# Attention work and weight splits rearranged over ACT, DVE and POOL in a fused attention and feed-forward kernel

## The chip, the cores and the metric

The kernel runs on one core of one Trainium2 chip. The metric is the device time of the whole program in microseconds (us), median of several runs; lower is better. The engines are named as the profile names them: PE (TensorE, matmuls), DVE (VectorE), ACT (ScalarE), POOL (GpSimd) and SP (SyncE, which here issues all DMAs).

## What is computed

Inputs are q, k, v of shape (4 batches, 8 heads, 576 tokens, 64 columns) and two pairs of weights, each w_in (512 x 2048) and w_out (2048 x 512), all fp32. The reference, cut to what matters:

```python
q_d, k_d, v_d = (t.reshape(B, H, S // 4, 4, D).mean(axis=3) for t in (q, k, v))
out_up = np.repeat(softmax(scale * q_d @ k_d.T) @ v_d, 4, axis=2)
mask = np.abs(pos[:, None] - pos[None, :]) < 4
out_local = softmax(np.where(mask, scale * q @ k.T, -1e9)) @ v
x = (out_up + out_local).transpose(0, 2, 1, 3).reshape(B * S, H * D)
h = x @ w_in1;  x = np.maximum(0.01 * h, h) @ w_out1       # 2304 tokens x 512
h = x @ w_in2;  out = (h - np.tanh(h)) @ w_out2
```

Both softmaxes subtract the row maximum and add 1e-9 to the row sum. The first attention works on means over four tokens ("downsampled"), the second only in a band of seven keys around each token ("local").

## The kernel before

**Matmuls.** Each fp32 matmul of the two feed-forward layers is done as three fp32r matmuls: an operand is split into a rounded part (`_hi`, a copy by ACT) and the rest (`_lo = raw - hi`, a subtraction by DVE or POOL), and hi*hi, hi*lo and lo*hi are summed in PSUM. All weights, all x and all g (the hidden activations) are split that way.

**Stages.** Heads are worked in 16 pairs. `batch0` computes the first four pairs (two in the buffers A, two in the buffers B) and four steps of the next. Then come eight tiles of layer 1 of 288 tokens each. The first six are "mixed": between the matmuls of a tile the engines do the steps of two more pairs of heads in the buffers A. The last two have layer 1 alone. Then follow six tiles of layer 2 of 384 tokens.

**Steps of a pair.** A pair takes 17 steps, one per slot. In batch0 pair A stands at step `slot % 17` and pair B five slots behind; in a mixed tile slot s runs step `(s + 4) % 17`. Steps 0 and 1: PE turns q, and the two halves are copied from PSUM into `q_diag` (ACT copies the one of step 0, DVE the one of step 1). Steps 2 and 3: the same for k into `kT`. Steps 3 and 4: DVE sums groups of four of both (the means). Steps 4 and 5: local scores, DVE adds the band. Step 5: POOL sums v over groups of four (`vd`, L970, three instructions), for which v must have been loaded. Step 6: DVE takes the local row maximum and subtracts it. Step 7: DVE takes the maximum of the downsampled scores (L814) and subtracts it (L816); ACT takes exp of the local scores (L588). Step 8: ACT takes exp of the downsampled scores `pd` (L591); DVE sums the local rows, adds 1e-9, inverts and multiplies `pl` by the inverse (L829). Step 9: DVE sums the downsampled rows (L835), adds 1e-9 and inverts. Step 10: POOL multiplies `pd` by the inverse (L977). Steps 11 to 14: PE turns `pl` and `pd`, ACT copies them out. Steps 15 and 16: PE multiplies with v, DVE combines both into xT (L765).

**Layer 1.** A tile runs over 16 chunks f of 128 hidden columns. PE computes `hidden1(f)`, then `down1(f - 2)`. ACT takes 0.01*h (L658), DVE the maximum (g, L871), ACT `g_hi` (L640), DVE `g_lo` (L856), and `down1(f)` waits for `g_lo(f)`. The weights of chunks 0 to 7 (`w_hi_a`, `w_lo_a`) are split once and kept: `split_kept(f)` is one ACT copy of 128 x 1024 (L616) and one POOL subtraction of the same size (L983). Before the change all eight are done in batch0, at the slots of `KEPT_SLOTS`. `hidden1(f)` waits for `kept_lo_done >= f + 1`. The weights of chunks 8 to 15 stay whole in `w_whole` and are split again in every tile (`in_hi`/`out_hi` by ACT, L624 and L628; `in_lo`/`out_lo` by POOL, L988 and L993). In the first tile of layer 1, ACT waits at chunk 6 for `whole_loaded`.

**Orders.** Every engine runs its own list of instructions in order. In batch0 the two pairs of a slot are sorted so that the one at a step under 6 comes first. In a mixed tile POOL's list for chunk f is `split_out(f-1)`, slot 2f, `split_in(f+2)`, slot 2f+1. ACT's is `split_out(f-1)`, leak(f), `g_hi(f-1)`, slot 2f, `split_in(f+2)`, slot 2f+1. DVE's is g(f), `g_lo(f-1)`, slot 2f, slot 2f+1. SP issues the loads in one order written out by hand, with waits in between: `load_qk(s, i)` waits for PE's step 3 of the pair before in the same buffers, `load_v(s, i)` for its step 16, `load_kept(f)` for `kept_lo_done >= f - 3`, since four slots of `w_whole` serve the kept weights in turn. The last four chunks of `w_whole` use the same four slots and are loaded when the kept ones there have been split.

Of the kernel before, what the change touches and what calls it, by code (L numbers as in the profile page):

```python
# [31 lines left out]
P = 128  # L32
# [8 lines left out]
KEPT_SLOTS = (9, 12, 17, 20, 25, 28, 33, 36)  # L41
# [16 lines left out]
def two_scale_attention_and_feed_forward(nc, q, k, v, w_in1, w_out1, w_in2, w_out2, out):  # L58
# [11 lines left out]
    SCALE = float(D) ** -0.5  # L70
    PAIRS = B * H // 2
# [9 lines left out]
    WHOLE = CF - KEPT  # L81
    assert D == QB and DM == CD * P and LP * RUN == S and NB * QB == S and PAIRS == 4 + 2 * MIXED

# [8 lines left out]
    with ExitStack() as ctx:  # L92
# [6 lines left out]
        def sem(name):  # L99
            return ctx.enter_context(nc.semaphore(name))  # L100
# [25 lines left out]
        class PairBuffers:  # L126

            def __init__(self, which, place, banks):
# [18 lines left out]
                self.exp_l, self.exp_d = sem(f"exp_l_{which}"), sem(f"exp_d_{which}")  # L147
                self.sum_l, self.sum_d = sem(f"sum_l_{which}"), sem(f"sum_d_{which}")
# [49 lines left out]
        whole_loaded = sem("whole_loaded")  # L198
# [19 lines left out]
        def uses0(i, n):  # L218


            return 7 * i + n
# [47 lines left out]
        def _(sp):  # L269
# [32 lines left out]
            def load_whole(j):  # L302
                if j >= WHOLE - 4:
                    sp.wait_ge(kept_lo_done, j - (WHOLE - 4) + KEPT - 3)
                load_w(w_whole[:, j, :], 0, KEPT + j, whole_loaded)
# [4 lines left out]
            load_kept(0)  # L310
            load_kept(1)
            load_qk(A, 1, 2)
            load_kept(2)
            load_kept(3)
            load_kept(4)
            load_qk(B, 1, 6)
            load_kept(5)
            load_v(A, 1, 2)
            load_kept(6)
            load_qk(A, 2, 8)  # L320
            load_kept(7)
            load_v(B, 1, 6)
            for j in range(WHOLE - 4):
                load_whole(j)
            load_v(A, 2, 8)
            for j in range(WHOLE - 4, WHOLE):
                load_whole(j)
            load_qk(A, 3, 10)
            load_v(A, 3, 10)
# [245 lines left out]
        def _(act):  # L575
            def attention(step, s, i):
                if step == 0:
                    act.wait_ge(s.bank_full[1], uses1(i, 1))
                    for h in range(2):
                        rows = slice(h * D, (h + 1) * D)  # L580
                        last = act.activation(q_part(s, rows, h, 0), token_part(s, rows, 0), ACT.Copy)
                    last.then_inc(s.bank_free[1], 1)
                elif step == 2:
                    act.wait_ge(s.bank_full[1], uses1(i, 2))
                    act.activation(k_part(s, 0), k_tokens(s, 0), ACT.Copy).then_inc(s.bank_free[1], 1)
                elif step == 7:
                    act.wait_ge(s.sub_l, i + 1)
                    act.activation(s.pl[:, :, :], s.pl[:, :, :], ACT.Exp, scale=SCALE).then_inc(s.exp_l, 1)  # L588
                elif step == 8:
                    act.wait_ge(s.bank_free[0], uses0(i, 4))  # L590
                    act.activation(s.pd[:, :, :], s.pd[:, :, :], ACT.Exp, scale=SCALE / FACTOR ** 2).then_inc(s.exp_d, 1)  # L591
# [26 lines left out]
            def split_in(tile, f):  # L618

                if f == KEPT:  # L620
                    act.wait_ge(whole_loaded, 32 * WHOLE)

                wait_from(act, h_done, CF * tile + (f - 1 if f >= KEPT + 2 else 0))
                act.activation(in_hi[:, f % 2, :], w_whole[:, f - KEPT, 0:DM], ACT.Copy).then_inc(in_hi_done, 1)  # L624
# [23 lines left out]
            def layer1(tile, between, extra, keep_before, ahead):  # L648
                for f in range(CF + 1):
                    n = CF * tile + f  # L650
                    if f == CF:
                        ahead()
                    if f - 1 >= KEPT:
                        split_out(tile, f - 1)
# [106 lines left out]
        def _(dve):  # L761
# [8 lines left out]
            def attention(step, s, i, batch, c):  # L770

                if step == 1:
                    dve.wait_ge(s.bank_full[0], uses0(i, 1))
                    for h in range(2):
                        rows = slice(h * D, (h + 1) * D)
                        last = dve.tensor_copy(q_part(s, rows, h, 1), token_part(s, rows, 1))
                    last.then_inc(s.bank_free[0], 1)
                elif step == 3:
                    dve.wait_ge(s.bank_full[0], uses0(i, 2))
                    dve.tensor_copy(k_part(s, 1), k_tokens(s, 1)).then_inc(s.bank_free[0], 1)  # L780

# [29 lines left out]
                elif step == 7:  # L811
                    dve.wait_ge(s.bank_full[0], uses0(i, 4))
                    quarter = s.banks[0:QP, 0, 0:QT * SD_].rearrange("p (t k) -> p t k", t=QT)
                    dve.tensor_reduce(s.mxd[:, :], quarter, AX_X, ALU.max).then_inc(s.max_d, 1)  # L814
                    dve.wait_ge(s.max_d, i + 1)
                    dve.tensor_tensor(s.pd[:, :, :], quarter,  # L816
                                      s.mxd[:, :].rearrange("p (t o) -> p t o", o=1).to_broadcast([QP, QT, SD_]),
                                      ALU.subtract).then_inc(s.bank_free[0], 1)
                elif step == 8:
# [8 lines left out]
                    dve.wait_ge(s.inv_l, i + 1)  # L828
                    dve.tensor_tensor(s.pl[:, :, :], s.pl[:, :, :],  # L829
                                      row_l.rearrange("p (n o) -> p n o", o=1).to_broadcast([P, NB, WIN]),  # L830
                                      ALU.mult).then_inc(s.norm_l, 1)
                elif step == 9:
                    row_d = s.rs[0:QP, NB:NB + QT]
                    dve.wait_ge(s.exp_d, i + 1)
                    dve.tensor_reduce(row_d, s.pd[:, :, :], AX_X, ALU.add).then_inc(s.sum_d, 1)  # L835
                    dve.wait_ge(s.sum_d, i + 1)
# [124 lines left out]
        def _(pool):  # L961
            def attention(step, s, i):
                if step == 5:
# [10 lines left out]
                    ins.then_inc(s.vd_done, 1)  # L974
                elif step == 10:
# [20 lines left out]
            def layer1(tile, between):  # L996
                for f in range(CF + 1):
                    if f - 1 >= KEPT:
                        split_out(tile, f - 1)
# [35 lines left out]
            hidden_score = -1e9 * float(D) ** 0.5  # L1035
# [56 lines left out]
```

## Time and profile before

| what | value |
|---|---|
| median of 3 runs | 1017.73 us (1016.67 to 1022.43) |
| span of the profiled execution | 1015.2 us |
| time of the profiled execution itself | not listed apart from its span |
| batch0 | from 0 to about 77 us |
| six mixed tiles | about 69.9 us each |
| mean granted clock of PE over the span | 0.986 |

A row of a timeline gives the start in us from the span's start, the duration in us, the engine, the line of the kernel, the operation, the tile written and the tiles read, the shape, the count, and in brackets how long the engine sat idle before and what ended that. Tiles of pair B stand in the trace under `xT` (as they lie in unused parts of it), `kT_b`, `qn_b`, `kn_b` and `acc`.

### The profile page before, as it was taken

Reading aid. Unit: us, or ns where it says so; the run is one execution under the profiler, and the core shown is the slowest. Engines: PE = TensorE matmul, PEld = TensorE weight load, DVE = VectorE, ACT = ScalarE, POOL = GpSimd, SP = SyncE. Lnnn points to the kernel's source line nnn. Section 1 sums busy time; section 2 is a strip of 40 time slices with the busy share of each in tenths; the row PEclk is TensorE's granted clock in tenths of the full one; section 3 lists DMA queues with packets and bytes.
Section 4 is the critical chain, followed back from the end, with each engine's and each line's share of the span. In section 5 each row is a group of like instructions: output and inputs, shape, how many; then the busy total and the mean of one; then the engine's idle time right before and its main releaser. Section 6 shows DMA issues by size and latency. Waiting matters only on the chain.

```text
span 1015.2 us, 19106 instructions
## 1 busy us (share of the span) xinstructions
PE 964.9 (95%) x6672; PEld 904.3 (89%) x6672; DVE 650.8 (64%) x1178; ACT 538.8 (53%) x1254; POOL 392.4 (39%) x325
## 2 busy tenths in 40 slices
PE   6679999999999999999999999999999999999997
PEld 6568989999899899899999998889899899898996
DVE  7775665864774676658423667677676676666764
ACT  2443443544534534435334667776575675766664
POOL 2651550631723515516234456633333233233232
PEclk9968999999999999999999999999999999999999
DMA  5863211121012012110100402200000000000000
GB/s 130 203 165 97 48 40 31 28 49 26 21 47 47 19 28 47 37 26 11 64 1 1 134 2 63 74 32 1 1 32 0 2 29 0 31 0 0 32 1 32
DMA packets 87221, 41.47 MB, mean 41 GB/s; under 512 B 59776, under 2 KB 80768, under 8 KB 87168
## 3 DMA queue, kind: packets, MB, share of 16 engines
q1 hardware_dynamic: 87168, 40.78, 15.2%
q8 instruction: 32, 0.52, 0.2%
q14 instruction: 21, 0.17, 0.1%
HBM read 36.04 MB, written 4.72 MB: 40 GB/s over the span
## 4 chain that ended last, share of the span: by engine, by line
PE 75%; DVE 9%; SPq 3%; ACT 3%; POOL 3%; issue 3%; DMA 3%; ACTq 0%; DVEq 0%
PE ph L458 12%; PE ph L460 11%; PE ph L459 11%; PE acc L534 6%; PE acc L535 6%; PE acc L536 6%; PE acc L487 6%; PE acc L489 5%; PE acc L488 5%; DVE g_lo L856 4%; PE banks L368 2%; PE banks L386 2%; POOL g_lo L1016 1%; POOL w_lo_b L1023 1%; DVE x_lo L851 1%
## 5 line engine op out<-in xcount | busy, mean ns | idle before, releaser
L1016 POOL TENSOR_TENSOR g_lo<-scratch,g_hi 128x384 fp32r<-128x384 f32 x96 | 126.0, 1312 | 258.9 <-ACT g_hi L640 258.9
L871 DVE TENSOR_TENSOR g<-g,ph 128x288 f32<-128x288 f32 x128 | 57.8, 452 | 161.1 <-ACT g L658 161.1
L988 POOL TENSOR_TENSOR in_lo<-w_whole,in_hi 128x512 fp32r<-128x512 f32 x64 | 88.0, 1375 | 177.2 <-ACT in_hi L624 177.2
L658 ACT ACTIVATE g<-ph 128x288 f32<-128x288 f32 x128 | 52.5, 410 | 192.1 <-PE ph L460 166.0
L458 PE MATMUL ph<-x_hi,w_hi_a 128*128 128x288 f32 (+1 forms) x448 | 144.9, 323 | 3.9 <-DVE x_lo L851 3.9
L460 PE MATMUL ph<-x_hi,w_lo_a 128*128 128x288 f32 (+1 forms) x448 | 140.6, 314 | 0.0
L459 PE MATMUL ph<-x_lo,w_hi_a 128*128 128x288 f32 (+1 forms) x448 | 140.5, 314 | 0.0
L907 DVE SCALAR_TENSOR_TENSOR scratch<-scratch,ph 128x384 f32<-128x384 f32 x96 | 53.2, 554 | 111.0 <-ACT scratch L703 106.4
L993 POOL TENSOR_TENSOR out_lo<-w_whole,out_hi 128x512 fp32r<-128x512 f32 x64 | 87.5, 1368 | 52.7 <-ACT out_hi L628 52.2
L702 ACT ACTIVATE scratch<-ph 128x384 f32<-128x384 f32 x96 | 46.8, 488 | 108.3 <-PE ph L460 106.8
L856 DVE TENSOR_TENSOR g_lo<-g,g_hi 128x288 fp32r<-128x288 f32 x128 | 100.0, 781 | 1.8 <-ACT g_hi L640 1.8
L487 PE MATMUL acc<-g_hi,out_hi 128*128 128x288 f32 x256 | 78.8, 308 | 13.8 <-DVE g_lo L856 13.7
L458 PEld LDWEIGHTS ph<-x_hi,w_hi_a 128*128 128x128 f32 x448 | 84.7, 189 | 8.0 <-issue 3.6
L459 PEld LDWEIGHTS ph<-x_lo,w_hi_a 128*128 128x128 f32 x448 | 84.8, 189 | 1.4
L460 PEld LDWEIGHTS ph<-x_hi,w_lo_a 128*128 128x128 f32 x448 | 84.8, 189 | 0.0
L458 PE MATMUL ph<-x_hi,in_hi 128*128 128x288 f32 x256 | 78.9, 308 | 0.0
L487 PE MATMUL acc<-g_hi,w_hi_a 128*128 128x288 f32 x256 | 78.7, 307 | 0.0
L489 PE MATMUL acc<-g_hi,out_lo 128*128 128x288 f32 x256 | 76.2, 298 | 0.0
L488 PE MATMUL acc<-g_lo,out_hi 128*128 128x288 f32 x256 | 76.0, 297 | 0.0
L459 PE MATMUL ph<-x_lo,in_hi 128*128 128x288 f32 x256 | 75.7, 296 | 0.0
L488 PE MATMUL acc<-g_lo,w_hi_a 128*128 128x288 f32 x256 | 75.6, 295 | 0.0
L489 PE MATMUL acc<-g_hi,w_lo_a 128*128 128x288 f32 x256 | 75.5, 295 | 0.0
(168 smaller groups left out, 2729.1 us busy)
## 6 DMA issues: line engine op xcount, KB each, us to landing
out_dram<-o_stage SPq DMA_DIRECT2D x18, 256.0 KB, 2.1
w_whole<-in_moe_w_in_dram SPq DMA_DIRECT2D x16, 256.0 KB, 4.5
w_whole<-in_moe_w_out_dram SPq DMA_DIRECT2D x16, 256.0 KB, 4.5
qn<-in_q_dram SPq DMA_DIRECT2D x28, 144.0 KB
kn<-in_k_dram SPq DMA_DIRECT2D x28, 144.0 KB
v4n<-in_v_dram SPq DMA_DIRECT2D x28, 144.0 KB
vw<-in_v_dram SPq DMA_DIRECT2D x28, 122.5 KB
scratch<-in_moe_w_in_dram SPq DMA_DIRECT2D x8, 256.0 KB, 3.0
```

Of the source, the lines that this page charges most:

```text
L458: pe.matmul(bank, whi, x_hi[:, c, 0:width], start=(c == 0), stop=False)
L459: pe.matmul(bank, whi, x_lo[:, c, 0:width], start=False, stop=False)
L460: last = pe.matmul(bank, wlo, x_hi[:, c, 0:width], start=False, stop=(c == CD - 1))
L487: pe.matmul(acc[:, c, 0:T1], whi, g1_hi[:, f % 3, :], start=(f == 0), stop=False)
L488: pe.matmul(acc[:, c, 0:T1], whi, g1_lo[:, f % 3, :], start=False, stop=False)
L489: last = pe.matmul(acc[:, c, 0:T1], wlo, g1_hi[:, f % 3, :], start=False, stop=(f == CF - 1))
L534: pe.matmul(acc[:, j, 0:DM], hi, whi, start=(f == 0), stop=False)
L535: pe.matmul(acc[:, j, 0:DM], hi, wlo, start=False, stop=False)
L856: dve.tensor_tensor(g1_lo[:, f % 3, :], g1[:, f % 2, :], g1_hi[:, f % 3, :].bitcast(F32), ALU.subtract).then_inc(g_lo_done, 1)
L988: pool.tensor_tensor(in_lo[:, f % 2, :], w_whole[:, f - KEPT, 0:DM], in_hi[:, f % 2, :].bitcast(F32), ALU.subtract).then_inc(in_lo_done, 1)
L993: pool.tensor_tensor(out_lo[:, f % 2, :], w_whole[:, f - KEPT, DM:CW], out_hi[:, f % 2, :].bitcast(F32), ALU.subtract).then_inc(out_lo_don ...
L1016: pool.tensor_tensor(g2_lo[:, f % 3, :], g2[:, f % 2, :], g2_hi[:, f % 3, :].bitcast(F32), ALU.subtract).then_inc(g_lo_done, 1)
```

## The change

Five edits, made together:

- `KEPT_SLOTS` shrinks from eight slots to (20, 25): batch0 does `split_kept` of chunks 0 and 1 only. Chunks 2 to 7 are done in the first tile of layer 1, by ACT and POOL, `split_kept(f + 2)` at the head of the list of chunk f, for f = 0 to 5.
- SP's order of loads changes: the q, k and v of the next pairs come ahead of weight loads, `kept(6)` and `kept(7)` behind the first four whole chunks, and the last four whole chunks behind q, k and v of pair A 3. They get a semaphore of their own (`rest_loaded`), for which ACT waits at chunk 10 of the first tile; `whole_loaded` now stands for the first four.
- ACT does all four copies of q and k; the scale is folded into them, and the exps and the hidden score change accordingly.
- The downsampled subtraction and row sums leave DVE: DVE takes the negated maximum, and ACT runs three exps of 96 x 144 straight from PSUM with it as bias, each with its row sum accumulated.
- The local normalisation (128 x 630) moves from DVE, step 8, to POOL, step 9.

```diff
-KEPT_SLOTS = (9, 12, 17, 20, 25, 28, 33, 36)
+KEPT_SLOTS = (20, 25)
...
+    Q_SCALE, K_SCALE = SCALE / FACTOR, 1.0 / FACTOR
+    L_SCALE = SCALE / (Q_SCALE * K_SCALE)
...
+    EARLY = len(KEPT_SLOTS)
...
-                load_w(w_whole[:, j, :], 0, KEPT + j, whole_loaded)
+                load_w(w_whole[:, j, :], 0, KEPT + j, whole_loaded if j < WHOLE - 4 else rest_loaded)
...
             load_kept(0)
+            load_qk(A, 1, 2)
             load_kept(1)
-            load_qk(A, 1, 2)
+            load_qk(B, 1, 6)
             load_kept(2)
+            load_v(A, 1, 2)
             load_kept(3)
+            load_v(B, 1, 6)
+            load_qk(A, 2, 8)
             load_kept(4)
-            load_qk(B, 1, 6)
             load_kept(5)
-            load_v(A, 1, 2)
-            load_kept(6)
-            load_qk(A, 2, 8)
-            load_kept(7)
-            load_v(B, 1, 6)
+            load_v(A, 2, 8)
             for j in range(WHOLE - 4):
                 load_whole(j)
-            load_v(A, 2, 8)
+            load_kept(6)
+            load_kept(7)
+            load_qk(A, 3, 10)
+            load_v(A, 3, 10)
             for j in range(WHOLE - 4, WHOLE):
                 load_whole(j)
-            load_qk(A, 3, 10)
-            load_v(A, 3, 10)
...
+                elif step == 1:
+                    act.wait_ge(s.bank_full[0], uses0(i, 1))
+                    for h in range(2):
+                        rows = slice(h * D, (h + 1) * D)
+                        last = act.activation(q_part(s, rows, h, 1), token_part(s, rows, 1), ACT.Copy, scale=Q_SCALE)
+                    last.then_inc(s.bank_free[0], 1)
...
+                elif step == 3:
+                    act.wait_ge(s.bank_full[0], uses0(i, 2))
+                    act.activation(k_part(s, 1), k_tokens(s, 1), ACT.Copy, scale=K_SCALE).then_inc(s.bank_free[0], 1)
...
-                    act.wait_ge(s.bank_free[0], uses0(i, 4))
-                    act.activation(s.pd[:, :, :], s.pd[:, :, :], ACT.Exp, scale=SCALE / FACTOR ** 2).then_inc(s.exp_d, 1)
+                    act.wait_ge(s.max_d, i + 1)
+                    for t in range(QT):
+                        last = act.activation(s.pd[:, t, :], s.banks[0:QP, 0, t * SD_:(t + 1) * SD_], ACT.Exp,
+                                              bias=s.mxd[:, t:t + 1], accum_out=s.rs[0:QP, NB + t:NB + t + 1])
+                    last.then_inc(s.bank_free[0], 1)
...
                 if f == KEPT:
-                    act.wait_ge(whole_loaded, 32 * WHOLE)
+                    act.wait_ge(whole_loaded, 32 * (WHOLE - 4))
+                if f == CF - 4:
+                    act.wait_ge(rest_loaded, 32 * 4)
...
+                    if isinstance(tile, int) and tile == 0 and EARLY <= f + 2 < KEPT:
+                        split_kept(f + 2)
...
-                    dve.tensor_reduce(s.mxd[:, :], quarter, AX_X, ALU.max).then_inc(s.max_d, 1)
-                    dve.wait_ge(s.max_d, i + 1)
-                    dve.tensor_tensor(s.pd[:, :, :], quarter,
-                                      s.mxd[:, :].rearrange("p (t o) -> p t o", o=1).to_broadcast([QP, QT, SD_]),
-                                      ALU.subtract).then_inc(s.bank_free[0], 1)
+                    dve.tensor_reduce(s.mxd[:, :], quarter, AX_X, ALU.max, negate=True).then_inc(s.max_d, 1)
...
-                    dve.wait_ge(s.inv_l, i + 1)
-                    dve.tensor_tensor(s.pl[:, :, :], s.pl[:, :, :],
-                                      row_l.rearrange("p (n o) -> p n o", o=1).to_broadcast([P, NB, WIN]),
-                                      ALU.mult).then_inc(s.norm_l, 1)
...
-                    dve.wait_ge(s.exp_d, i + 1)
-                    dve.tensor_reduce(row_d, s.pd[:, :, :], AX_X, ALU.add).then_inc(s.sum_d, 1)
-                    dve.wait_ge(s.sum_d, i + 1)
+                    dve.wait_ge(s.bank_free[0], uses0(i, 4))
...
+                elif step == 9:
+                    pool.wait_ge(s.inv_l, i + 1)
+                    pool.tensor_tensor(s.pl[:, :, :], s.pl[:, :, :],
+                                       s.rs[:, 0:NB].rearrange("p (n o) -> p n o", o=1).to_broadcast([P, NB, WIN]),
+                                       ALU.mult).then_inc(s.norm_l, 1)
...
+                    if isinstance(tile, int) and tile == 0 and EARLY <= f + 2 < KEPT:
+                        split_kept(f + 2)
...
-            hidden_score = -1e9 * float(D) ** 0.5
+            hidden_score = -1e9 / L_SCALE
```

The DVE copies of q and k (steps 1 and 3 there) go out. Layer 2, the two unmixed tiles and PE's own list stay as they were.

## Rows read from the trace of the kernel before

**Rows 1.** The page's first part: PE's busy time, share of the span, instructions.

```profile
PE 964.9 (95%) x6672; PEld 904.3 (89%) x6672; DVE 650.8 (64%) x1178; ACT 538.8 (53%) x1254; POOL 392.4 (39%) x325
```

**Rows 2.** Windows over the first, second and last mixed tile: length, busy by engine, PEclk, DMA.

```profile
76.00:147.00 71.00, 66.68 (x571) 64.60 (x568) 43.00 (x79) 31.52 (x77) 26.21 (x23) 0.96 0.25 61
147.00:217.00 70.00, 67.56 (x585) 65.34 (x584) 45.53 (x84) 31.77 (x78) 27.47 (x24) 1.00 0.15 36
...
427.00:497.00 70.00, 67.56 (x568) 65.37 (x567) 44.94 (x83) 30.41 (x74) 27.29 (x24) 0.98 0.11 28
```

**Rows 3.** Timeline of SP's DMA queue in batch0: start, time to issue.

```profile
16.75 3.20 SPq L291 DMA_DIRECT2D xT<-in_v_dram  x1
...
37.38 0.81 SPq L282 DMA_DIRECT2D v4n<-in_v_dram  x1
...
45.66 1.64 SPq L273 DMA_DIRECT2D qn<-in_q_dram  x2
...
50.22 0.34 SPq L282 DMA_DIRECT2D xT<-in_v_dram  x1
...
52.34 3.77 SPq L291 DMA_DIRECT2D xT<-in_v_dram  x1
```

**Rows 4.** Timeline of POOL in batch0.

```profile
26.48 2.35 POOL L983 TENSOR_TENSOR w_lo_a<-w_whole,w_hi_a 128x1024 fp32r<-128x1024 f32 x1 [6.48 <-ACT w_hi_a L616]
28.80 2.31 POOL L970 TENSOR_TENSOR xT<-xT 72x256 f32<-72x256 f32 x3
...
60.02 2.32 POOL L970 TENSOR_TENSOR xT<-xT 72x256 f32<-72x256 f32 x3 [5.74 <-DMA xT<-in_v_dram]
62.30 0.90 POOL L977 TENSOR_TENSOR pd<-pd,rs 96x432 f32<-96x432 f32 x1
63.16 2.35 POOL L983 TENSOR_TENSOR w_lo_a<-w_whole,w_hi_a 128x1024 fp32r<-128x1024 f32 x1
```

**Rows 5.** Timeline of DVE in batch0: a local normalisation, and the last combine.

```profile
61.93 4.26 DVE L829 TENSOR_TENSOR xT<-xT 128x630 f32<-128x630 f32 x1
...
76.39 0.69 DVE L765 TENSOR_TENSOR xT<-acc,xT 128x512 f32<-128x512 f32 x1 [0.95 <-PE acc L386]
```

**Rows 6.** Groups by line and shape, whole span: count, busy us, mean ns, idle before.

```profile
L983 POOL TENSOR_TENSOR w_lo_a<-w_whole,w_hi_a 128x1024 fp32r<-128x1024 f32 x8 | 18.9, 2360 | 16.1 <-ACT w_hi_a L616 16.1
...
L776 DVE COPY q_diag<-banks 64x288 f32<-64x288 f32 x28 | 12.7, 454 | 11.3 <-PE banks L362 11.1
L977 POOL TENSOR_TENSOR pd<-pd,rs 96x432 f32<-96x432 f32 x14 | 12.7, 906 | 74.8 <-DVE rs L839 74.8
...
L816 DVE TENSOR_TENSOR pd<-banks,mxd 96x432 f32<-96x432 f32 x14 | 8.4, 603 | 0.5
L616 ACT ACTIVATE w_hi_a<-w_whole 128x1024 fp32r<-128x1024 f32 x8 | 8.4, 1052 | 6.7 <-DMA w_whole<-in_moe_w_out_dram 6.7
...
L611 ACT ACTIVATE up<-banks 128x144 f32<-128x144 f32 x14 | 4.1, 292 | 13.2 <-PE banks L394 12.6
```

**Rows 7.** Timelines of PE and DVE in the first mixed tile.

```profile
90.85 0.29 PE L487 MATMUL acc<-g_hi,w_hi_a 128*128 128x288 f32 x1
...
94.83 0.38 PE L487 MATMUL acc<-g_hi,w_hi_a 128*128 128x288 f32 x1
...
91.52 0.82 DVE L829 TENSOR_TENSOR pl<-pl,rs 128x630 f32<-128x630 f32 x1
```

**Rows 8.** Timelines of DVE, POOL and PE late in the second mixed tile.

```profile
194.81 1.95 DVE L829 TENSOR_TENSOR pl<-pl,rs 128x630 f32<-128x630 f32 x1
...
199.43 4.71 DVE L856 TENSOR_TENSOR g_lo<-g,g_hi 128x288 fp32r<-128x288 f32 x1
...
196.04 1.86 POOL L988 TENSOR_TENSOR in_lo<-w_whole,in_hi 128x512 fp32r<-128x512 f32 x1
...
202.57 1.25 POOL L993 TENSOR_TENSOR out_lo<-w_whole,out_hi 128x512 fp32r<-128x512 f32 x1
...
204.29 0.37 PE L487 MATMUL acc<-g_hi,out_hi 128*128 128x288 f32 x1 [1.71 <-DVE g_lo L856]
```

More of the change, by code:

```diff
@@ L146, in __init__ @@
                 self.means_done, self.sub_l = sem(f"means_done_{which}"), sem(f"sub_l_{which}")
-                self.exp_l, self.exp_d = sem(f"exp_l_{which}"), sem(f"exp_d_{which}")
-                self.sum_l, self.sum_d = sem(f"sum_l_{which}"), sem(f"sum_d_{which}")
+                self.exp_l, self.sum_l = sem(f"exp_l_{which}"), sem(f"sum_l_{which}")
                 self.eps_l, self.eps_d = sem(f"eps_l_{which}"), sem(f"eps_d_{which}")
@@ L580, in attention @@
                         rows = slice(h * D, (h + 1) * D)
-                        last = act.activation(q_part(s, rows, h, 0), token_part(s, rows, 0), ACT.Copy)
+                        last = act.activation(q_part(s, rows, h, 0), token_part(s, rows, 0), ACT.Copy, scale=Q_SCALE)
                     last.then_inc(s.bank_free[1], 1)
+                elif step == 1:
[4 more added lines that the diff above has]
+                    last.then_inc(s.bank_free[0], 1)
                 elif step == 2:
                     act.wait_ge(s.bank_full[1], uses1(i, 2))
-                    act.activation(k_part(s, 0), k_tokens(s, 0), ACT.Copy).then_inc(s.bank_free[1], 1)
+                    act.activation(k_part(s, 0), k_tokens(s, 0), ACT.Copy, scale=K_SCALE).then_inc(s.bank_free[1], 1)
+                elif step == 3:
+                    act.wait_ge(s.bank_full[0], uses0(i, 2))
+                    act.activation(k_part(s, 1), k_tokens(s, 1), ACT.Copy, scale=K_SCALE).then_inc(s.bank_free[0], 1)
                 elif step == 7:
                     act.wait_ge(s.sub_l, i + 1)
-                    act.activation(s.pl[:, :, :], s.pl[:, :, :], ACT.Exp, scale=SCALE).then_inc(s.exp_l, 1)
+                    act.activation(s.pl[:, :, :], s.pl[:, :, :], ACT.Exp, scale=L_SCALE).then_inc(s.exp_l, 1)
                 elif step == 8:
-                    act.wait_ge(s.bank_free[0], uses0(i, 4))
-                    act.activation(s.pd[:, :, :], s.pd[:, :, :], ACT.Exp, scale=SCALE / FACTOR ** 2).then_inc(s.exp_d, 1)
+                    act.wait_ge(s.max_d, i + 1)
[3 more added lines that the diff above has]
+                    last.then_inc(s.bank_free[0], 1)
                 elif step == 11:
@@ L770, in attention @@
             def attention(step, s, i, batch, c):
[L772 to L780, printed above, removed]
+                if step == 3:
                     dve.wait_ge(s.bank_free[1], uses1(i, 1))
```

2 lines of the change are left out of this document (1 added, 1 removed).

## The prediction

> **What bounds the kernel now.** I read the page first: PE is busy 95% of the span [rows 1], so time can only come from places where PE is not fed, and the rest of the chip matters where it feeds PE. Then the windows by stage. A mixed tile lasts 70 us and PE is busy 67.56 of them [rows 2]; 2.4 us a tile is nearly all there is to win in these six. The two unmixed tiles and layer 2 are not touched by the change. That leaves batch0, the stage before the first tile, where PE has little work and a chain through all engines sets the pace; it ends with the last combine, at 76.39 + 0.69 us [rows 5]. Then the timelines. In batch0 the reader should look at what POOL waits for: at 26.48 it has stood 6.48 us for a weight split behind ACT, which itself waited for weights from DRAM, and the sum of v (L970) that stands behind it in POOL's list starts only at 28.80; at 60.02 it has stood 5.74 us for v of pair B 1 [rows 4]. In the late mixed tile the reader should look at two durations: `g_lo` took 4.71 us, and PE stood 1.71 us for it [rows 8].
>
> The second point carries most of what follows. Uncontended, DVE's 128x630 product of two SBUF operands takes 0.82 us [rows 7]. At 194.81 it took 1.95 and ended when a POOL instruction had ended; POOL's next one (196.04) then took 1.86 for its usual 1.3, as it waited in its turn [rows 8]. The `g_lo` that started at 199.43 ended 0.3 us after POOL's instruction of 202.57 to 203.82, and in batch0 the one of 61.93 took 4.26 and ended 0.7 us after POOL's weight split of 63.16 to 65.51 [rows 4, 5, 8]. So such a DVE instruction and a POOL instruction exclude each other, and a POOL queue whose instructions are all ready is not interrupted: DVE waits for the queue, not for one instruction. DVE instructions that read PSUM (L816, the copies) show no such wait.
>
> The Trainium skill (SBUF — State Buffer, section "Who interferes with whom") says that a DVE instruction with two SBUF inputs contends with a POOL instruction that reads SBUF, and that the loser blocks until the first has finished. The trace agrees with the exclusion; the 4.71 us goes past one instruction, where by the page's rule it would be 1.7 at most. What that rule would do to the time is the first rival.
>
> **Part 1, batch0.** Removed there: six of eight weight splits, 2.36 us of POOL and 1.05 of ACT each [rows 6]. On the path is the one of 26.48. With it gone the v sum of pair B 0 waits only for its load: issued until 16.75 + 3.20 = 19.95, and landing as the later one did, 60.02 - (52.34 + 3.77) = 3.9 us after the issue [rows 3, 4], so at 23.9 instead of 28.8. That is -4.9; I take -4.4, because the POOL normalisation comes in. PE's step 16 of pair A 0, and SP's load of v of A 1 at 37.38 that waits for it [rows 3], come earlier by that. Next, v of B 1: before, SP issues v of A 1, kept(6), q and k of A 2, kept(7), and gets to it at 50.22, 12.84 us after 37.38. Now only v of A 1 and kept(3) stand between, which take what v of A 1 and kept(6) took, 45.66 - 37.38 = 8.3 us [rows 3]. That is another -4.5, -9 in all at 60.02. POOL's `pd` product at 62.30 follows, and from it the chain to the combine at 76.39 is copies and transposes: 14 us, as before. Two ACT splits of 1.05 leave it, and a second q and k copy (0.454 each for 288 columns on DVE [rows 6], and there are three a pair, which ACT now does one after the other) come in: -2.1 + 1.4, about -0.5. The DVE work removed (per pair three copies of 0.454, the subtraction of 0.603 [rows 6], a sum of about the same, the product of 0.82 [rows 7]: 3.4 us) shortens a busy engine, but the v of B 1 is then what is late, so I count nothing more for it. Sum: **-9.4**, bounds -4 (only the first wait goes; the rest comes back on the chain through ACT) and -13 (the removed DVE work of one pair shows too).
>
> **Part 2, the first tile.** The six splits land on POOL and ACT while PE is fed by DVE. ACT's copy for weight chunk 4 stands ahead of leak(2), and POOL's 2.36 us then run just when `g_lo(1)` is due; PE wanted it at 90.85 [rows 7]. ACT's 1.05 is also ahead of it: PE waits about 2.5 us. Behind `g_lo(1)` DVE sums and inverts the local rows, about 1.3 us; POOL multiplies, 1.3 to 1.45 us (0.906 x 630/432 by the `pd` product, 2.36 x 630/1024 by the split [rows 6]), where DVE took 0.82; PE's turn of `pl` waits another 1.2. Then POOL's queue has no hole: product 1.4, split 5 2.36, `pd` 0.91, split 6 2.36, together 7.0 us [rows 6], and `g_lo(2)` asks for its turn in it. PE, now 3.7 late, wants it at 94.83 + 3.7 = 98.5 [rows 7] and gets it near 101.5: 3 more. Sum 6.7, and I take **+6** as ACT runs a little ahead in places; bounds +2.5 (only the first wait) and +10 (with a fall of the clock, below). SP's part: kept(6) and kept(7) are issued once splits 2 and 3 are done, some 15 us before their use; the last whole chunks are issued after v of A 3, whose wait ends near chunk 6, and need about 4 us for v, 5.5 for the four loads and 3.9 to land, while chunk 10 comes some 18 us later. I cost both at nothing; the margin is about 4 us.
>
> **Part 3, the rest of the mixed tiles.** Per tile: in the first half POOL's product takes 0.5 to 0.6 more than DVE's 0.82 and PE's turn stands right behind it; after some slack +0.3 (bounds 0, +0.6). In the second half the DVE instruction of 194.81 goes and POOL gets 1.4 us between its splits. POOL's queue at 194.8 then runs without a hole through `out_lo`, the product and `in_lo` (4.0 us), so `g_lo(10)` comes about 0.8 later than now, and the next, that of 199.43 [rows 8], meets the same queue of `pd`, `out_lo`, `in_lo`, `out_lo`. It comes out between 1.0 earlier, if the last of these loses its turn because ACT is late with its copy, and 0.3 later. At the tile's end ACT's second q copy (2 x 0.45) delays `x_hi` by about 1 us, while the later `out_lo` leaves `x_lo` alone: 0 to +0.2. I take +0.3 a tile, times 6: **+2**, bounds -4 and +14. The three exps of 144 columns cost ACT 3 x 0.292 = 0.9 [rows 6] for one exp of about 0.6; it lies beside POOL and PE work. Of these I know no row with a row sum accumulated; at twice the price, 1.8, `leak(11)` and with it `g_lo(10)` would come 0.9 later.
>
> **Sum.** -9.4 + 6 + 2 = -1.4 us, made against the span of 1015.2; the median of the runs is 2.5 above that span, and I carry the difference over: 1017.7 - 1.4 = **1016.3**. What a measurement of this kernel can tell from no change is 0.5%, 5.1 us.
>
> **Clock.** The first tile's window has a mean clock of 0.96 and the last one's 0.98 [rows 2]: 0.02 x 70 is 1.4 us, one short fall to half (1.2 GHz) after the wait for `g_lo`, absent in the second tile with the same wait. Part 2's waits are longer, so one or two such falls are likely there, 1.4 us each at least; this is in the bounds, not in the sum.
>
> **Rivals.**
> (a) DVE gets its turn after each POOL instruction, as at 194.81 [rows 8]. Then part 2 is +2.5 and part 3 about -0.4 a tile, -2.5: -9.4 + 2.5 - 2.5 gives 1008.3. For it: that row, and the skill's rule named above. Against it: 4.71 and 4.26 us. Chance 0.32 (with a batch0 gain at its upper bound beside it).
> (b) Slower: in each mixed tile ACT's k copy (0.45) delays `in_hi(10)`, POOL's v sums slip, and `in_lo(11)` is then ready before they end, so that POOL runs `in_lo` and `out_lo` on without letting `g_lo(8)` in, 2.6 us more; all behind it slips, and PE loses about 2 a tile. Six tiles: -9.4 + 6 + 14 gives 1028. It decides from 1.1 us a tile on. Against it: the three v sums wait for each other, a hole in which DVE can enter. Chance 0.16.
> (c) Batch0 gives 4, not 9: its end is set by copies in a row on ACT, not by loads. -4 + 6 + 2 gives 1021.7. Chance 0.08.
> (d) The last weights come late, and ACT stands at chunk 10: 5 us past the margin would give 1021. Chance 0.04.
> The forecast itself: 0.40, own range 1012.7 to 1022.5.
>
> Faster by over 0.5%: (a) and a little of the forecast, 0.34. Within: the rest of the forecast, (c) and (d) nearly whole, 0.46. Slower: (b) and the edge of (c) and the forecast, 0.20. The range, 1006 to 1026, leaves out most of (b) and the far end of (a).
>
> **What the profile after would show.** Batch0's last combine at 67 +/- 2, POOL's v sums near 24 and 51. In the first tile waits of PE (L487) on DVE `g_lo` at chunks 3 and 4, of 2.5 and 3 us, with DVE instructions of 2.5 and 6 us beside a closed row of POOL instructions. In the second tile PE's idle time within 1 us of 2.4, again at `g_lo`. Wrong if: a mixed tile changes by over 1 us, if batch0 ends after 73, or if PE stands for `kept_lo` or ACT for a load.

## The result, and the profile after

The changed kernel takes 1002.15 us (median of 4 runs, 1001.27 to 1004.44), the one before 1017.4 beside it (4 runs): ratio 0.984 [0.982, 0.986], 1.6% faster. The prediction was 1016.3 with a range from 1006 to 1026, so the time lies 4 us under the range. The profiled execution's span fell from 1015.2 to 999.6 us.

The page's first part after answers to [rows 1]:

```profile
PE 965.1 (97%) x6672; PEld 906.1 (91%) x6672; DVE 585.8 (59%) x1082; ACT 565.8 (57%) x1382; POOL 410.4 (41%) x341
```

PE's work is the same; it stands idle 15.8 us less (34.5 for 50.3 of the span). To see where, I cut both traces at the first DVE `x_lo` of every tile, where a tile starts. Before, these are at 78.0, 146.7, 216.6, 286.5, 356.5, 426.4 and 495.8, after at 71.2, 141.3, 209.9, 278.3, 346.7, 415.1 and 480.8:

| stretch | before | after | difference |
|---|---|---|---|
| up to the first tile | 78.0 | 71.2 | -6.8 |
| first mixed tile | 68.7 | 70.1 | +1.4 |
| second to fifth, each | 69.9 | 68.4 to 68.6 | -5.9 in all |
| sixth | 69.4 | 65.8 | -3.6 |
| all the rest | 519.4 | 518.8 | -0.6 |

Windows cut at these points, over the first, second and sixth tile, first of the kernel before and then of the kernel after (columns as in [rows 2]):

```profile
78.00:146.70 68.70, 66.02 (x561) 64.13 (x562) 42.00 (x77) 30.73 (x75) 24.75 (x21) 0.97 0.23 54
146.70:216.60 69.90, 67.47 (x584) 65.24 (x584) 45.43 (x82) 31.67 (x77) 27.47 (x24) 1.00 0.15 36
...
426.40:495.80 69.40, 66.96 (x564) 64.83 (x563) 44.34 (x81) 29.81 (x72) 27.48 (x24) 0.98 0.10 23
```

```profile
71.20:141.30 70.10, 66.53 (x564) 64.56 (x565) 38.92 (x66) 38.40 (x93) 42.48 (x31) 0.98 0.39 106
141.30:209.90 68.60, 67.32 (x586) 65.36 (x585) 36.34 (x71) 35.24 (x93) 29.58 (x26) 1.00 0.15 36
...
415.10:480.80 65.70, 64.71 (x560) 62.71 (x559) 36.14 (x70) 33.23 (x89) 29.71 (x26) 1.00 0.10 25
```

The timeline of POOL in batch0 after, which answers to [rows 4]:

```profile
23.67 2.71 POOL L969 TENSOR_TENSOR xT<-xT 72x256 f32<-72x256 f32 x3 [2.90 <-DMA xT<-in_v_dram]
...
50.45 2.35 POOL L987 TENSOR_TENSOR w_lo_a<-w_whole,w_hi_a 128x1024 fp32r<-128x1024 f32 x1 [5.81 <-ACT w_hi_a L630]
53.16 1.24 POOL L976 TENSOR_TENSOR pl<-pl,rs 128x630 f32<-128x630 f32 x1 [0.36 <-DVE rs L832]
54.36 2.32 POOL L969 TENSOR_TENSOR xT<-xT 72x256 f32<-72x256 f32 x3
```

The first v sum starts at 23.67, where 23.9 was forecast, and for its load alone. The second starts at 54.36 instead of 60.02, where 51 was forecast: it stands behind a weight split that came at 50.45, and behind the new product. That product waited for DVE, and the timeline of DVE shows why, together with the last combine ([rows 5]):

```profile
50.51 2.32 DVE L830 TENSOR_SCALAR rs<-rs 128x9 f32<-128x9 f32 x1
...
69.92 0.69 DVE L783 TENSOR_TENSOR xT<-acc,xT 128x512 f32<-128x512 f32 x1 [0.37 <-PE acc L388]
```

An addition on nine numbers a partition takes 2.32 us: it ends as the split ends, at 52.8. The last combine ends at 69.92 + 0.69 = 70.61, where 67 was forecast.

In the first tile the timelines of PE, POOL and DVE after answer to [rows 7]:

```profile
86.60 0.40 PE L489 MATMUL acc<-g_hi,w_hi_a 128*128 128x288 f32 x1 [2.32 <-DVE g_lo L855]
...
89.10 0.63 PE L376 MATMUL banks<-ident,pl 128*70 128x128 f32 x4 [0.64 <-POOL pl L976]
```

```profile
87.80 1.24 POOL L976 TENSOR_TENSOR pl<-pl,rs 128x630 f32<-128x630 f32 x1 [1.57 <-DVE rs L832]
89.00 2.61 POOL L987 TENSOR_TENSOR w_lo_a<-w_whole,w_hi_a 128x1024 fp32r<-128x1024 f32 x1
91.57 0.90 POOL L981 TENSOR_TENSOR pd<-pd,rs 96x432 f32<-96x432 f32 x1
92.43 2.39 POOL L987 TENSOR_TENSOR w_lo_a<-w_whole,w_hi_a 128x1024 fp32r<-128x1024 f32 x1
95.35 2.38 POOL L987 TENSOR_TENSOR w_lo_a<-w_whole,w_hi_a 128x1024 fp32r<-128x1024 f32 x1 [0.53 <-ACT w_hi_a L630]
```

```profile
84.49 2.05 DVE L855 TENSOR_TENSOR g_lo<-g,g_hi 128x288 fp32r<-128x288 f32 x1
...
88.21 1.14 DVE L855 TENSOR_TENSOR g_lo<-g,g_hi 128x288 fp32r<-128x288 f32 x1
...
92.17 2.97 DVE L855 TENSOR_TENSOR g_lo<-g,g_hi 128x288 fp32r<-128x288 f32 x1
```

POOL's row of instructions without a hole is there, from 87.80 to 94.82: product, split, `pd`, split, as forecast. But the `g_lo` that asks at 88.21, inside the product, has ended at 89.35: it went in as the product ended, and the split behind took 2.61 for 2.35. The `g_lo` that asks at 92.17, inside `pd`, comes out only at 95.14, 0.3 us after the queue ran empty. One row, two behaviours.

Late in the second tile, DVE and POOL after ([rows 8] is the same place before):

```profile
190.41 0.99 DVE L855 TENSOR_TENSOR g_lo<-g,g_hi 128x288 fp32r<-128x288 f32 x1
...
193.40 0.66 DVE L855 TENSOR_TENSOR g_lo<-g,g_hi 128x288 fp32r<-128x288 f32 x1
```

```profile
191.04 1.46 POOL L976 TENSOR_TENSOR pl<-pl,rs 128x630 f32<-128x630 f32 x1
192.46 1.28 POOL L992 TENSOR_TENSOR in_lo<-w_whole,in_hi 128x512 fp32r<-128x512 f32 x1
193.69 1.13 POOL L981 TENSOR_TENSOR pd<-pd,rs 96x432 f32<-96x432 f32 x1
194.79 1.28 POOL L997 TENSOR_TENSOR out_lo<-w_whole,out_hi 128x512 fp32r<-128x512 f32 x1
```

The `g_lo` of 4.71 us is now one of 0.66. It asks at 193.40, 0.3 us ahead of `pd` and inside `in_lo`; before, it asked at 199.43, 0.2 us behind the start of `pd` (199.21). PE's waits of 0.39 and 1.71 us for `g_lo` are gone from tiles 2 to 6. Two smaller ones have come in each of these tiles, here in the PE timeline of the third:

```profile
212.97 0.40 PE L489 MATMUL acc<-g_hi,out_hi 128*128 128x288 f32 x1 [0.71 <-DVE g_lo L855]
...
225.87 0.30 PE L376 MATMUL banks<-ident,pl 128*70 128x128 f32 x1 [0.33 <-POOL pl L976]
```

The first has taken the place of a wait of 0.33 for `x_lo`. 0.39 + 1.71 + 0.33 before less 0.71 + 0.33 after is 1.39 a tile; the tiles are 1.3 to 1.5 shorter.

### The profile page after: what moved, and what is told of

It is laid out like the page before. It is cut to its first block, busy times and chain, and to the rows that moved or that the text cites. A ratio compares the mean times of both kernels' runs of the same rounds, so it can differ in the third digit from the quotient of the medians.

```text
span 999.6 us, 19154 instructions
## 1 busy us (share of the span) xinstructions
PE 965.1 (97%) x6672; PEld 906.1 (91%) x6672; DVE 585.8 (59%) x1082; ACT 565.8 (57%) x1382; POOL 410.4 (41%) x341
## 4 chain that ended last, share of the span: by engine, by line
PE 84%; DVE 5%; ACT 4%; POOL 2%; issue 2%; SPq 2%; DMA 1%; ACTq 0%; DVEq 0%
PE ph L460 12%; PE ph L462 12%; PE ph L461 12%; PE acc L536 6%; PE acc L537 6%; PE acc L538 6%; PE acc L489 6%; PE acc L490 6%; PE acc L491 6%; PE banks L370 3%; PE banks L388 2%; DVE g_lo L855 2%; PE banks L376 2%; PE banks L364 1%; PE banks L396 1%
## 5 line engine op out<-in xcount | busy, mean ns | idle before, releaser
L992 POOL TENSOR_TENSOR in_lo<-w_whole,in_hi 128x512 fp32r<-128x512 f32 x64 | 83.4, 1304 | 161.7 <-ACT in_hi L640 161.1
L855 DVE TENSOR_TENSOR g_lo<-g,g_hi 128x288 fp32r<-128x288 f32 x128 | 88.0, 687 | 2.7 <-ACT g_hi L656 2.7
L460 PE MATMUL ph<-x_hi,in_hi 128*128 128x288 f32 x256 | 78.5, 307 | 0.0
```

Of the source, the lines that this page charges most:

```text
L460: pe.matmul(bank, whi, x_hi[:, c, 0:width], start=(c == 0), stop=False)
L855: dve.tensor_tensor(g1_lo[:, f % 3, :], g1[:, f % 2, :], g1_hi[:, f % 3, :].bitcast(F32), ALU.subtract).then_inc(g_lo_done, 1)
L992: pool.tensor_tensor(in_lo[:, f % 2, :], w_whole[:, f - KEPT, 0:DM], in_hi[:, f % 2, :].bitcast(F32), ALU.subtract).then_inc(in_lo_done, 1)
```

## The experiments

A is the splits moved into the first tile with the new order of loads, B all copies of q and k on ACT, C the three exps, D the local normalisation on POOL. Where B is absent, DVE's copies are multiplications by the same scale. "Steady tile" is the length of tiles 2 to 5, "start" the first `x_lo`, both of one profiled execution a kernel. The stretches given for the kernel before are always those of its one kept profile, with a span of 1015.2 us; the medians beside them were taken anew with each group of runs and differ (1017.4 to 1020.5). So what the stretches add up to is not what the medians differ by: for A, 6.2 us of span against 9.5 us of median.

### Each part alone

A is `KEPT_SLOTS` with the splits in the first tile, the loads and the semaphore for the last of them; of the rest of the diff above it has only the folded scales, as all kernels of this section made from the changed one do. B, C and D in short, against the kernel before:

```diff
 # B: steps 1 and 3 leave DVE
+                elif step == 1:
...
+                        last = act.activation(q_part(s, rows, h, 1), token_part(s, rows, 1), ACT.Copy, scale=Q_SCALE)
...
+                elif step == 3:
...
+                    act.activation(k_part(s, 1), k_tokens(s, 1), ACT.Copy, scale=K_SCALE).then_inc(s.bank_free[0], 1)
 # C: step 8
+                    for t in range(QT):
+                        last = act.activation(s.pd[:, t, :], s.banks[0:QP, 0, t * SD_:(t + 1) * SD_], ACT.Exp,
+                                              bias=s.mxd[:, t:t + 1], accum_out=s.rs[0:QP, NB + t:NB + t + 1])
 # D: step 8 on DVE becomes step 9 on POOL
+                    pool.tensor_tensor(s.pl[:, :, :], s.pl[:, :, :], ...
```

A: 

> The kernel before with part A alone: six of the eight weight splits in the first tile, the new order of loads; DVE keeps its copies, its downsampled shift and sum, and its local normalisation (the scales are folded into the copies as in the changed kernel, which changes no time). Theory 1 (the steady tiles won because work left DVE): the steady tiles stay at 69.9 us, the opening ends 5 to 7 us earlier, the first tile pays 3 or more; 1012 to 1016 in all. Theory 2 (the gain came mostly with the order of loads and splits): 1008 or less. The rule of the prediction (a closed POOL queue is never interrupted) would have the first tile pay about 6: 1014.

B: 

> The kernel before with part B alone: ACT takes all four q and k copies. Theory 1: DVE's order changes only at the tile's end and in its middle, x_lo no longer waits behind the q copy; steady tile 69.5 to 70.2, time within 3 us of before. Theory 3 (ACT's longer list is what shifts POOL's splits and breaks up the collision): steady tile 68.5 or less, time down by 7 or more.

C: 

> The kernel before with part C alone: ACT runs three exps from PSUM with bias and accumulated sums, DVE loses the subtraction and the sum (1.2 us a pair). Theory 1: the inverse of the local rows is ready 0.6 us earlier and DVE's product at the late chunks of a tile meets POOL's queue elsewhere; steady tile 69 to 70, opening 1 to 2 us shorter, time down by 2 to 6. Rival: the accumulate makes each exp dearer and ACT's list later: same or up to 3 slower.

D: 

> The kernel before with part D alone: the local normalisation on POOL. Theory 1 (the product on DVE is what pushed the late g_lo into the closed POOL queue): the g_lo of 4.7 us is gone, steady tile 68.2 to 68.8, time down by 6 to 9, though PE then waits 0.3 us a tile for POOL's product. The rule of the prediction: steady tile 70.2, time up by 2.

| kernel | median us | ratio [95%] | start | first tile | steady tile |
|---|---|---|---|---|---|
| before | 1020.5 | 1 | 78.0 | 68.7 | 69.9 |
| A | 1011.05 | 0.992 [0.990, 0.995] | 67.8 | 75.3 | 69.9 |
| B | 1022.47 | 1.001 [0.999, 1.004] | 80.8 | 69.5 | 70.1 |
| C | 1012.84 | 0.992 [0.990, 0.995] | 79.4 | 68.4 | 69.1 to 69.2 |
| D | 1005.21 | 0.987 [0.983, 0.990] | 78.5 | 67.1 | 68.1 |

D alone gives most of the gain, in the place where the prediction gave it a small loss. A alone does what parts 1 and 2 of the prediction had it do, -10.2 and +6.5. B gives nothing that can be told from noise. D's median is 15.3 us under the one before, where its theory 1 said 6 to 9 and the prediction's rule +2; C's is 7.7 under, where 2 to 6 was expected. DVE in D, late in the second tile, beside POOL:

```profile
197.79 0.68 DVE L859 TENSOR_TENSOR g_lo<-g,g_hi 128x288 fp32r<-128x288 f32 x1
```

```profile
195.44 1.46 POOL L980 TENSOR_TENSOR pl<-pl,rs 128x630 f32<-128x630 f32 x1
196.86 1.28 POOL L996 TENSOR_TENSOR in_lo<-w_whole,in_hi 128x512 fp32r<-128x512 f32 x1
198.11 1.12 POOL L985 TENSOR_TENSOR pd<-pd,rs 96x432 f32<-96x432 f32 x1
```

The `g_lo` now stands ahead of `pd`. From this I formed the theory that the next runs try: what shuts DVE out of POOL's whole queue is a POOL instruction on fewer than 128 partitions (`pd` has 96, the v sums 72) with the next one ready behind it; behind one on 128 partitions DVE is let in. The second half of it turned out to need a condition, which stands at the end of the section on 112 partitions.

### The product of pd on 128 partitions

The kernel before, with the product widened over 32 more partitions of ones, which nothing reads. POOL's instructions keep their order and count; DVE sets the ones with four instructions more at the start of the program:

```diff
-                    pool.tensor_tensor(s.pd[:, :, :], s.pd[:, :, :],
+                    pool.tensor_tensor(s.pd_all[:, :, :], s.pd_all[:, :, :],
...
-                                       .to_broadcast([QP, QT, SD_]), ALU.mult).then_inc(s.norm_d, 1)
+                                       .to_broadcast([P, QT, SD_]), ALU.mult).then_inc(s.norm_d, 1)
```

> The kernel before with one thing changed: POOL's product of pd and its inverse (step 10) covers all 128 partitions instead of 96; the 32 more rows hold ones and are read by nobody. Theory S (skew): an instruction on 96 partitions leaves part of POOL's eight cores free to begin the next one, and from then on there is no moment between POOL's instructions in which DVE gets in; with 128 partitions there is. Then the g_lo that starts beside the late pd product takes 1.0 to 1.4 us instead of 4.7, PE's wait of 1.7 behind it goes, and a steady tile takes 68.2; time down by 8 to 12. Theory R (readiness, the rule of the prediction: a POOL queue that is ready is not interrupted): g_lo still takes 4.7, steady tile 69.9, time as before.

1006.32 against 1019.25 us, ratio 0.988 [0.984, 0.992], steady tile 68.0. DVE and POOL at the place of [rows 8]:

```profile
201.64 1.00 DVE L857 TENSOR_TENSOR g_lo<-g,g_hi 128x288 fp32r<-128x288 f32 x1
```

```profile
201.42 0.91 POOL L980 TENSOR_TENSOR pd<-pd,rs 128x432 f32<-128x432 f32 x1 [1.31 <-DVE rs L840]
202.28 1.51 POOL L996 TENSOR_TENSOR out_lo<-w_whole,out_hi 128x512 fp32r<-128x512 f32 x1
```

`g_lo` asks 0.22 us behind the start of `pd`, as before, with `out_lo`, `in_lo` and `out_lo` in a row behind it, as before, and takes 1.00 us for 4.71. `out_lo` takes 1.51 for 1.28, as it waits for its turn. PE's wait of 1.71 is gone. The product itself costs no more (0.91 for 0.906). The median is 12.9 us lower, a little more than the 8 to 12 expected.

### 112 partitions, and a wait behind 96

The first has the product on 112 partitions instead of 128 (`[112, QT, SD_]`). The second leaves it on 96, and POOL waits for its own end before it goes on:

```diff
                                        .to_broadcast([QP, QT, SD_]), ALU.mult).then_inc(s.norm_d, 1)
+                    pool.wait_ge(s.norm_d, i + 1)
```

112 partitions: 

> As the run on 128 partitions, but POOL's product of pd covers 112, the 16 more rows again ones that nobody reads. Theory S in its sharp form (one core of POOL that is free early is enough): g_lo takes 4.7 us again, steady tile 69.9, time as before. If only the number of rows or their place matters: between, 68.0 to 69.9.

The wait: 

> The kernel before with one wait more: POOL waits for its own pd product (96 partitions) to complete before it goes on. Theory S: all of POOL's cores stand for a moment, DVE gets in, g_lo takes about 1.0 to 1.1, steady tile 68.0 to 68.2, time down by 10 to 14, as with 128 partitions. Rival (something in the 128-partition instruction itself, not the skew between the cores): g_lo 4.7, time as before.

112 partitions: 1020.14 against 1017.85 us, ratio 1.001 [1.000, 1.003]; PE's wait stays at 1.72, and the steady tile at 69.9 (71.4 in the two of them in which the granted clock fell to its lower level for 3.4 us). The wait: 1007.37, ratio 0.989 [0.987, 0.992], steady tile 68.0. DVE's rows, first of the one with 112 partitions, then of the one with the wait, and POOL's of the latter:

```profile
200.40 4.71 DVE L857 TENSOR_TENSOR g_lo<-g,g_hi 128x288 fp32r<-128x288 f32 x1
```

```profile
201.33 1.00 DVE L856 TENSOR_TENSOR g_lo<-g,g_hi 128x288 fp32r<-128x288 f32 x1
```

```profile
201.11 0.90 POOL L977 TENSOR_TENSOR pd<-pd,rs 96x432 f32<-96x432 f32 x1 [1.31 <-DVE rs L839]
202.09 1.38 POOL L994 TENSOR_TENSOR out_lo<-w_whole,out_hi 128x512 fp32r<-128x512 f32 x1
```

So it is neither the place, nor the amount of work, nor `pd` as such: 96 and 112 partitions shut DVE out, 128 don't, and 96 don't either once POOL's next instruction can't start before the product has wholly ended. That costs POOL some 0.1 us (0.98 us from start to start, 0.87 before).

The other kept traces narrow the rule down in two ways. First, a POOL instruction on 128 partitions does not let DVE in when the row that it stands in began, without a hole, with one on fewer. In the second tile after, the third v sum (72 partitions) ends at 183.40, `in_lo` has been ready since ACT's copy ended at 182.64, and DVE asks at 184.10, inside `in_lo`:

```profile
181.75 1.65 POOL L969 TENSOR_TENSOR vd<-vd,v4n 72x256 f32<-72x256 f32 x2
183.36 1.27 POOL L992 TENSOR_TENSOR in_lo<-w_whole,in_hi 128x512 fp32r<-128x512 f32 x1
184.59 1.28 POOL L997 TENSOR_TENSOR out_lo<-w_whole,out_hi 128x512 fp32r<-128x512 f32 x1
```

```profile
182.02 0.62 ACT L640 ACTIVATE in_hi<-w_whole 128x512 fp32r<-128x512 f32 x1
```

```profile
184.10 2.45 DVE L817 TENSOR_TENSOR pl<-pl,mxl 128x630 f32<-128x630 f32 x1
```

DVE gets nothing at the end of `in_lo` (184.63), only at the end of `out_lo` (185.87), and its 0.82 us become 2.45; so in all 18 mixed tiles of the three kernels that have B (the whole change, B alone, and B with C and D). Second, the next instruction has to be ready early enough. `g_lo` asks 60 times during a third v sum on 72 partitions with `in_lo` right behind it. In 58 of them ACT's copy for `in_lo` ended 0.11 to 0.22 us before the end of the v sum, and DVE was let in at that end; in two it ended 0.23 us before, and `g_lo` was shut out until the queue was empty, as here in the sixth tile of A, C and D:

```profile
458.30 3.48 DVE L855 TENSOR_TENSOR g_lo<-g,g_hi 128x288 fp32r<-128x288 f32 x1
```

Against these, `g_lo` asks 187 times in the 13 traces during a POOL instruction on 128 partitions with another right behind it, in rows that had no such beginning, and is let in at its end every time.

### Three parts, and two

```diff
 # no A: the kernel after, with the kernel before's slots and loads
-KEPT_SLOTS = (20, 25)
+KEPT_SLOTS = (9, 12, 17, 20, 25, 28, 33, 36)
 # no B: the kernel after, with steps 1 and 3 back on DVE
+                    dve.tensor_scalar(k_part(s, 1), k_tokens(s, 1), K_SCALE, None, ALU.mult).then_inc(s.bank_free[0], 1)
 # A and D: no B, and DVE's subtraction and sum instead of the three exps
```

B, C and D: 

> The changed kernel without part A (eight splits in the opening and the old order of loads). Alone A gave 10 us in the opening and paid 6.5 in the first tile. If the opening is bound by its loads and the splits, it ends at 78 to 80 and the time is 1005 to 1008; if C and D have already taken what A took, it ends at 74 to 76 and the time is near 1003.

A, C and D: 

> The changed kernel without part B (DVE has its q and k copies back, with the scale in them). If B costs what it cost alone (opening +3, steady tile +0.25), the opening ends at 68, the steady tile takes 68.1, and the time is 4 to 6 below the changed kernel, 996 to 998. If B's copies matter only in an opening bound by DVE, which A, C and D relieve, it is within 2 of the changed kernel.

A and D: 

> Parts A and D alone (splits and loads moved, local normalisation on POOL). Opening near 68, steady tile 68.1 as with D alone. The first tile paid 6.5 us with A alone; by the prediction's row of POOL instructions (product, split, pd, split without a hole) it pays at least as much here, 73 to 75, and the time is 998 to 1001. By theory S the product on 128 partitions leaves DVE a way in, so the first tile takes 70 to 72 and the time is 996 to 998.

| kernel | median us | ratio [95%] | start | first tile | steady tile |
|---|---|---|---|---|---|
| B, C, D | 1010.24 | 0.993 [0.990, 0.995] | 81.6 | 67.3 | 68.4 |
| A, C, D | 999.82 | 0.982 [0.979, 0.985] | 73.3 | 72.0 | 68.1 |
| A, D | 999.81 | 0.982 [0.979, 0.985] | 69.9 | 71.3 | 68.1 to 68.2 |

A and D alone give at least what all four do. B costs 0.3 us in a steady tile (68.4 with it, 68.1 without): the wait of 0.71, where without B there is one of 0.33. The two medians without B are 2.3 under the whole change, each taken against its own kernel before; with ratios of 0.982 and 0.984 and their intervals, a gain of the whole kernel from leaving B out is not shown. For A, C and D, 996 to 998 was expected if B costs what it costs alone, and else within 2 of the whole change: 999.82 is 2.3 under it. For A and D theory S named 996 to 998 and a first tile of 70 to 72: the tile came (71.3), the time did not (999.81). The ratios of the parts alone would add up to 2.7%, the whole gives 1.6%: the wait of 0.39 that C takes away is one of the two that D takes away, and A's gain of 10.2 in batch0 is 8.1 beside D and 6.8 in the whole change, each in one profile; which part takes it is not shown. For B, C and D, 1005 to 1008 was expected and a start at 78 to 80; 1010.24 and 81.6 were measured, and why is open.

### A better version

A and D, with four splits in batch0 instead of two, and the product of `pd` on 128 partitions:

```diff
-KEPT_SLOTS = (20, 25)
+KEPT_SLOTS = (20, 25, 28, 33)
```

> A better kernel, built from what the runs showed: parts A and D, four weight splits in the opening (slots 20, 25, 28, 33) and four in the first tile instead of two and six, and the pd product on 128 partitions. Against parts A and D alone (999.8): the first tile loses its wait of 1.9 for g_lo at chunk 3 if the split of chunk 4 is the first there, or keeps it, as that split still stands ahead of leak(2); steady tile 67.9 to 68.1. Time 996 to 1000. If the two more splits lengthen the opening by their 2.4 us each, 1002.

997.96 us, ratio 0.983 [0.979, 0.986]; start 66.4, first tile 71.7, steady tile 68.1. Its median is under those of all other kernels here, but its interval holds those of A with D and of the whole change: a version that is better than the changed one by a measurable amount is not shown. PE still waits 1.92 and 0.64 us in the first tile, so the two splits more in batch0 did not spare these waits. The start came earlier with more work in batch0 (66.4 for 69.9). Its profile has 20.5 us at the lower clock there and that of A with D has 34.1, but whether this is the reason is not shown.

## Why the prediction was wrong

**The rule on the closed queue (failed; the cause is shown).** The prediction had that "a POOL queue whose instructions are all ready is not interrupted: DVE waits for the queue, not for one instruction". It drew this from two rows, 4.71 and 4.26 us, and left the 1.95 us of [rows 8] to rival (a). Both rows have a POOL instruction on fewer than 128 partitions at the point where DVE asks: `pd` for the one, the v sums on 72 and then `pd` for the other. The row of 1.95 asks during `out_lo` on 128 and is let in at its end, ahead of `in_lo`. The runs with 128 and 112 partitions and with the wait settle it. The Trainium skill (GPSIMD Engine Reference, section "Instruction dispatch") has that the partitions are split among GpSimd's cores by 16, each core taking the instructions from the queue by itself. That agrees with the runs: cores without a share would already be in the next instruction when the others end, so that there is no moment in which POOL as a whole has let go. By that picture the cores stay apart through the rest of the row, and the next instruction has to be there before the others end, as the rows of 2.45 and 3.48 us have it. The inner picture is argued all the same; the dependence on 128 partitions and on the wait is shown by runs, the two conditions by rows alone.

**Part 3, forecast +2, measured -5.9 in tiles 2 to 5 and -3.6 in the sixth (the largest miss).** The step was that `g_lo` of 199.43 "meets the same queue". D puts a product on 128 partitions into POOL's list and frees DVE of 1.95 us; `pd` waits behind `in_lo`, and `g_lo` asks during `in_lo`, whose end lets it in. -1.4 a tile where +0.3 was taken; 1.7 a tile over five tiles is 8.5 of the 14 us by which the prediction was off. In the sixth tile a fall of the clock comes on top: before, the granted clock is 0.98 there (3.4 us at the lower level), after, 1.00. A alone, which has the same late waits as the kernel before and no such fall, takes 67.8 for that tile, so the fall is worth some 1.5 of the 3.6. The prediction's own sign of being wrong, a mixed tile that changes by over 1 us, had come. Two smaller terms of part 3 were right: the product 0.4 to 0.6 longer on POOL with PE's turn 0.33 late (+0.3 forecast), and B's second copies at the tile's end +0.3 to +0.4 (0 to +0.2 forecast). Rival (a), that DVE gets its turn after each POOL instruction, had the right sign and -0.4 a tile; it too missed that the 4.71 us would go, as it let the same meeting stand.

**Part 2, forecast +6, measured +1.4.** The first two terms, 2.5 and 1.2, came as 2.32 and 0.64. The third, 3 us for PE's wait on `g_lo(2)` in the closed row, did not come at all: that `g_lo` took 1.14 us and PE did not wait, by the same failed rule. The later one of 2.97 us cost PE nothing either. Against them stand the two waits of 0.39 and 1.70 late in that tile before, which went. PE's waits over the tile went from 4.32 to 4.87 us (both with the one for `x_lo`), its busy time from 66.02 to 66.53: +1.1 of the +1.4. In A alone, with those late waits still there, the tile is 6.5 longer, close to the +6. But there the sum fits by luck: 3.1 of it are waits (1.92 and 1.52, less 0.33 at the tile's start), and 3.1 are busy time at a lower granted clock, 0.94 over that tile where it was 0.97, which the sum had left out. The last weights came in time: ACT waits for no load in that tile.

**Part 1, forecast -9.4, measured -6.8.** A alone gives -10.2, so the working on the loads held: there the first v sum starts at 23.35, and the second at 49.35, as its load lands (51 was forecast):

```profile
49.35 2.37 POOL L977 TENSOR_TENSOR xT<-xT 72x256 f32<-72x256 f32 x3 [0.94 <-DMA xT<-in_v_dram]
```

The two halves of A, fewer splits and the order of loads, were not run apart. In the whole change the second v sum is at 54.36. What stands ahead of it are the split of 50.45, the product of 1.24 (forecast 1.3 to 1.45), and DVE's 2.32 us behind that split; the prediction had asked only what DVE loses, not what POOL's new product would be late for. The load itself was also later: SP had issued it by 47.99, in A alone by 45.53.

**The clock in batch0** stays open. The granted clock is at its lower level (1.2 GHz) for parts of every batch0, between 2.4 us (C alone) and 46.1 us (`pd` on 128 partitions) of it in single profiles; A, C and D have 41.6. The starts of the kernels, 66 to 82 us, are moved by it in a way that one profile a kernel doesn't separate from the edits. How far it can move them is seen where batch0 is all but the same: the kernel before, the one with `pd` on 128 partitions, the one with 112 and the one with the wait have 20.1, 46.1, 43.7 and 10.4 us at the lower level and start at 78.0, 80.3, 78.7 and 78.7. The page's row of the clock, before and then in A, C and D, 25 us a digit:

```profile
PEclk9968999999999999999999999999999999999999
```

```profile
PEclk9558999999999999999999999999999999999999
```

**C** costs ACT 1.2 us for three exps with their sums (0.9 forecast, 1.8 feared), and PE's waits for `g_lo` became no longer by it: with C alone the one of 0.39 is gone and the one of 1.71 is 1.60.

**The sum.** Against the forecast, part 1 came out 2.6 us worse, part 2 4.6 better, part 3 11.5 better (-9.5 for +2), and the rest of the span 0.6 better: 14.1 in all. The 2.5 us by which the prediction puts the median above the span joins different executions: after the change the profiled one took 1001.37 us, 1.8 above its own span of 999.6. The forecast is a change, so this moves nothing.

## What to carry to other kernels

When a DVE instruction in SBUF is several times longer than usual, look not only at what POOL does at its start but back along POOL's row to the last hole. If an instruction on fewer than 128 partitions stands in that row with its successor ready behind it, widen it or let POOL wait for its end; here either was worth 1.1 to 1.2%, the wait with one line. A stall that depends on who asks first, by 0.2 us, can vanish by any edit near it, so price its disappearance as a case of its own before adding tenths. And measure the parts alone: two of the four, A and D, carried the whole gain.

## What the hardware showed that I had not expected

- A `g_lo` of 128x288 takes 0.45 us alone, 1.00 when it asks during a POOL product on 128 partitions, and 4.71 when it asks during the same product on 96 or 112 with three ready instructions behind. An instruction on 128 partitions does not let DVE in either, if such a one stands ahead of it without a hole (0.82 us became 2.45).
- The POOL product of 432 elements takes 0.91 us on 96, 112 and 128 partitions alike.
- DVE's small fp32 additions in SBUF contend too: 128x9 took 0.17 us alone and 2.32 behind a split, 96x3 took 0.17 alone and 1.20 behind a product.
- An ACT exp of 96x144 with a row sum is an instruction of 0.36 to 0.38 us and a second one of 0.20 that reads the sum; the next exp starts 0.35 us after the one before.
